# Weight splits moved from VectorE to GpSimd, with earlier refills and earlier high halves, in a linear attention and expert MLP kernel

## What is computed

```python
# attention, for every step t of every batch and head
y[:, :, t] = einsum('bhd,bhde->bhe', rt, state + (u * kt) outer vt)
state = wt[:, :, :, None] * state + kt outer vt
# MLP
h = maximum(x @ w_in, 0.0)
x = h * h @ w_out
# experts: tokens with x @ w_skip > 0 go to the expert with the highest logit
h = maximum(xc[mask] @ w1[e], 0.0)
y[mask] = gate_w[mask, None] * (h @ w2[e])
out[do_compute] = xc + y
```

## Time and profile before

| | us |
|---|---|
| median of 3 runs | 793.04 (792.3 to 793.43) |
| the profiled execution, its own time | 793.43 |
| its span | 791.7 |
| PE busy in the span | 759.2 |
| DVE / ACT / POOL busy | 468.3 / 323.9 / 224.9 |
| PE's chunk 0 in the trace | about 42.6 to 137.8 |

### The profile page before, as it was taken

How to read it: one execution, slowest core, us unless ns; L and a number is a source line. 1 busy time by engine, 2 the same in 40 slices (tenths; PEclk the granted TensorE clock), 3 DMA queues, 4 the chain that set the end, 5 groups by cost and what they waited for, 6 DMA issues and landing times.

```text
span 791.7 us, 15634 instructions
## 1 busy us (share of the span) xinstructions
PE 759.2 (96%) x5571; PEld 661.7 (84%) x5571; DVE 468.3 (59%) x755; ACT 323.9 (41%) x636; POOL 224.9 (28%) x215
## 2 busy tenths in 40 slices
PE   6699999999999999999999999999999999999994
PEld 3478788888888888888888889898889998999984
DVE  7876877766676665866576744344442246443861
ACT  3463443533344334433343333253342355353841
POOL 7842423222234220511242220253421002212210
PEclk9899999999999999999999999999999999999998
DMA  9874222422233223322231105155662116616520
GB/s 231 243 226 164 47 60 64 140 49 61 61 102 91 61 61 101 91 60 60 55 115 49 37 32 200 42 171 176 208 224 69 61 61 211 210 61 223 195 76 7
DMA packets 50420, 88.19 MB, mean 111 GB/s; under 512 B 5949, under 2 KB 33833, under 8 KB 50353
## 3 DMA queue, kind: packets, MB, share of 16 engines
q1 hardware_dynamic: 42192, 62.19, 28.1%
q0 software_dynamic: 7584, 24.31, 8.4%
q10 hardware_dynamic: 576, 0.79, 0.3%
HBM read 72.98 MB, written 16.75 MB: 113 GB/s over the span
## 4 chain that ended last, share of the span: by engine, by line
PE 82%; DVE 6%; DMA 4%; ACT 3%; issue 2%; POOL 1%; SPq 1%; DVEq 0%; POOLq 0%; ACTq 0%
PE bank L600 24%; PE bank L602 22%; PE bank L601 22%; DMA work<-sorted_rows 3%; PE bank L654 3%; PE bank L864 2%; PE bank L699 2%; PE bank L683 2%; ACT spare L968 1%; DMA work<-rkw 1%; PE bank L723 1%; PE bank L663 1%; PE bank L811 1%; DVE hid L1370 1%; DVE spare L1202 1%
## 5 line engine op out<-in xcount | busy, mean ns | idle before, releaser
L600 PE MATMUL bank<-wo_hi,h_hi 128*128 128x394 f32 (+1 forms) x576 | 201.8, 350 | 1.0 <-DVE h_lo L1491 1.0
L602 PE MATMUL bank<-wo_hi,h_lo 128*128 128x394 f32 (+1 forms) x576 | 196.6, 341 | 0.0
L601 PE MATMUL bank<-wo_lo,h_hi 128*128 128x394 f32 (+1 forms) x576 | 196.0, 340 | 0.0
L1370 DVE SCALAR_TENSOR_TENSOR hid<-bank,hid 128x512 f32<-128x512 f32 x96 | 65.1, 678 | 137.7 <-ACT hid L1011 137.7
L1011 ACT ACTIVATE hid<-bank 128x512 f32<-128x512 f32 x96 | 57.1, 594 | 158.0 <-PE bank L602 157.7
L600 PE MATMUL bank<-xt_hi,wi_hi 128*128 128x512 f32 x288 | 117.9, 409 | 0.1
L600 PEld LDWEIGHTS bank<-wo_hi,h_hi 128*128 128x128 f32 x576 | 108.7, 189 | 6.6 <-DVE h_lo L1491 1.2
L602 PE MATMUL bank<-xt_hi,wi_lo 128*128 128x512 f32 x288 | 112.9, 392 | 0.0
L601 PE MATMUL bank<-xt_lo,wi_hi 128*128 128x512 f32 x288 | 112.7, 391 | 0.0
L601 PEld LDWEIGHTS bank<-wo_lo,h_hi 128*128 128x128 f32 x576 | 108.8, 189 | 2.9
L602 PEld LDWEIGHTS bank<-wo_hi,h_lo 128*128 128x128 f32 x576 | 108.7, 189 | 0.0
(11 more groups left out here) (152 smaller groups left out, 1219.2 us busy)
## 6 DMA issues: line engine op xcount, KB each, us to landing
work<-rkw SPq DMA_DIRECT2D x48, 192.0 KB, 3.8
spare<-rk_rows SPq DMA_DIRECT2D x22, 384.0 KB, 4.2
work<-v_rows SPq DMA_DIRECT2D x25, 192.0 KB, 3.8
work<-sorted_rows SPq DMA_DIRECT2D x24, 193.0 KB, 2.6
work<-rkw SPq DMA_DIRECT2D x48, 96.0 KB, 3.3
x_cur<-sorted_rows SPq DMA_DIRECT2D x24, 192.0 KB, 2.4
work<-w POOLq DMA_DIRECT2D x6, 768.0 KB, 6.7
x<-w POOLq DMA_DIRECT2D x6, 768.0 KB, 9.7
```

Source lines behind the costliest of these rows:

```text
L600: pe.matmul(ps, a_hi, b_hi, start=start, stop=False, skip_group_check=True)
L601: pe.matmul(ps, a_hi, b_lo, start=False, stop=False, skip_group_check=True)
L602: return pe.matmul(ps, a_lo, b_hi, start=False, stop=stop, skip_group_check=True)
L1370: dve.scalar_tensor_tensor(hid[:, f % 2, :], HID[f % 2][:, :], 0.0, hid[:, f % 2, :], ALU.max, ALU.mult).then_inc(sb_sq, 1)
```

## The change

It has four parts. `keep_decay` moves from ACT to DVE, behind the scan that it reads, and the scans of units 2 to 4 no longer wait for it. The low halves of pieces 3 to 7 move from DVE to POOL: pieces 3 and 4 behind the factors of unit (1, 1), 5 and 6 behind those of (1, 2), 7 behind those of (1, 3). ACT's high halves of pieces 5, 6 and 7 stand one block earlier, at f = 6, 8 and 10. On SP, `refill(1, 2)` goes ahead of piece 6, and `refill(1, 3)` ahead of piece 7.

```diff
--- before.py
+++ after.py
@@ -281,7 +281,7 @@
         ROUTE_STEPS = 16
         LATE = 6
         SHORT = 7
-        SPLITS_AT = (1, 3, 5, 7, 9, 11)
+        SPLITS_AT = (1, 3, 5, 6, 8, 10)
         CHOICE_SLOT = 4
         GATE_SLOT = 12
         RANKS_UNIT = 2
@@ -499,11 +499,11 @@
             load_mlp_piece(4)
             load_transposed(2)
             load_mlp_piece(5)
+            refill(1, 2)
             load_mlp_piece(6)
             load_transposed(3)
+            refill(1, 3)
             load_mlp_piece(7)
-            refill(1, 2)
-            refill(1, 3)
             refill(2, 0)
             refill(2, 1)
             save_x2(0, 0)
@@ -1067,20 +1067,10 @@
                 act.wait_ge(ps_wg_turned, n + 1)
                 act.activation(wo_hi[:, 4 * n:4 * n + 4, DM:], gate_columns(n), ACT.Copy).then_inc(wg_hi, 1)
 
-            def keep_decay(b):
-
-                act.wait_ge(cum_done, b + 1)
-                act.activation(last_decay[0:PK, b, :].unsqueeze(2), by_time(cum[b % 2])[0:PK, :, T:T + 1], ACT.Copy
-                               ).then_inc(decay_saved, 1)
-
-            keep_decay(0)
             own_diagonal(0, 0)
-            keep_decay(1)
             for b in range(B):
                 if b == 1:
                     split_hi(0)
-                if b == 1 or b == 2:
-                    keep_decay(b + 1)
                 if b == 3:
                     take_gate(0)
                 take_k(0, b)
@@ -1175,10 +1165,14 @@
                     dve.wait_ge(r_done, unit - 1)
                 if not (isinstance(c, int) and unit <= B):
                     dve.wait_ge(sb_state, unit - 1)
-                elif unit >= 2:
-                    dve.wait_ge(decay_saved, unit - 1)
                 dve.tensor_tensor_scan(cum[n][0:PK], w_dec[n][0:PK], start_col[0:PK, :], 0.0,
                                        ALU.mult, ALU.add).then_inc(cum_done, 1)
+
+            def keep_decay(b):
+
+                dve.wait_ge(cum_done, b + 1)
+                dve.tensor_copy(last_decay[0:PK, b, :].unsqueeze(2), by_time(cum[b % 2])[0:PK, :, T:T + 1]
+                                ).then_inc(decay_saved, 1)
 
             def inverse(c, b, part):
 
@@ -1396,20 +1390,11 @@
                 dve.tensor_tensor(wo_lo[:, 4 * n:4 * n + 4, DM:], gate_columns(n),
                                   wo_hi[:, 4 * n:4 * n + 4, DM:].bitcast(F32), ALU.subtract).then_inc(wg_lo, 1)
 
-            def split_lo(k):
-
-                raw, hi, lo = mlp_piece(k)
-                dve.wait_ge(w_hi, k + 1)
-                dve.wait_ge(w_lo, k)
-                dve.tensor_tensor(lo, raw, hi.bitcast(F32), ALU.subtract).then_inc(w_lo, 1)
-
             def chunk(i, par, c, cg, c_last=False, late=0, per=8):
                 for f in range(NF):
                     square(i, f)
                     side(2 * f - late, c, cg, par, c_last, per)
                     square_lo(i, f)
-                    if isinstance(i, int) and i == 0 and f in SPLITS_AT[1:]:
-                        split_lo(2 + SPLITS_AT.index(f))
                     side(2 * f + 1 - late, c, cg, par, c_last, per)
                 for n in range(2 * NF - late, 2 * NF):
                     side(n, c, cg, par, c_last, per)
@@ -1437,9 +1422,11 @@
                 inverse(c, b, 1)
 
             decays(0, 0)
+            keep_decay(0)
             inverses(0, 0)
             own_term(0, 0)
             decays(0, 1)
+            keep_decay(1)
             inverse(0, 1, 0)
             mask_scores(0, 0, 0)
             mask_scores(0, 0, 1)
@@ -1448,6 +1435,7 @@
             for b in range(2):
                 take_xlo(0, 0, b)
                 decays(0, b + 2)
+                keep_decay(b + 2)
                 inverse(0, b + 2, 0)
                 mask_scores(0, b + 1, 0)
                 mask_scores(0, b + 1, 1)
@@ -1690,8 +1678,14 @@
             split_lo(1)
             keys(1, 0)
             split_lo(2)
-            for b in range(1, B):
-                factors(1, b)
+            factors(1, 1)
+            for k in (3, 4):
+                split_lo(k)
+            factors(1, 2)
+            for k in (5, 6):
+                split_lo(k)
+            factors(1, 3)
+            split_lo(7)
             for b in range(B):
                 factors(2, b)
```

## The result

The changed kernel takes **807.15 us** (median of 4 runs, 805.11 to 808.68), beside 793.23 us for the kernel before (4 runs, 792.3 to 793.77): a ratio of **1.0175, 95% interval [1.015, 1.02]**. It is slower, as forecast, but by 13.9 us instead of 5.1, and it lies 6 us above the top of the range. Run again on another chip it took 807.27 us. The profiled execution took 806.28 us, with a span of 804.6 us where before had 791.7.

What follows compares the result with a forecast made beforehand. PE, busy 759.2 of 791.7 us, was taken as the bound. Stall 3.9, removed wait -0.7, clock 1.7 and copies 0.2 sum to +5.1 us, giving 798.1 us; range 793.4 to 801.0.

Steps and rivals of the forecast that it cites:

- the delay beside POOL: Chunk 0, blocks 8 to 9: POOL's splits delay one DVE operation before `sb_state` by 0.8 us; bounds none and two.
- the clock: After PE's long wait before `k_transpose` of unit (1, 2), the granted clock falls once, costing 1.7 us; bounds 0 and 1.7.
- the step that carries the shift at the end of chunk 0 unchanged to the end: From chunk 1 on PE hardly waits, so chunk 0's shift reaches the kernel's end; nothing added later.
- The main term of the prediction: End of chunk 0: late piece 7 holds up ACT, moving `k_transpose` of unit (1, 2) 3.9 us later, from 105.35 to 109.3.
- Piece 6 and the other moves: Piece 6 lands at about 85.8, costing nothing; other moved halves cost nothing; `keep_decay` copies on DVE cost 0.2 us.
- the wait of 0.66 us at 115.35: PE's wait for `xt_lo` of unit (1, 2) in chunk 0 goes with DVE's split at 111.39, saving 0.7 us.
- What POOL adds: Chunk 0: low halves fit POOL's idle time but delay DVE once, 0.8 us, so `sb_state` reaches 6 at 96.3, not 95.5.
- This wait of 1.63 us goes: Chunk 0: without DVE's split at 86.52, `xt_lo` of unit (1, 1) is ready before PE arrives at 91.9.
- The new wait: Chunk 0: piece 7, issued at 99.0 behind `refill(1, 3)`, lands at 105.2; PE idles 6.4 us, `k_transpose` starts at 109.3.
- the mark of an error in its frame: Stated sign: the prediction is wrong in its frame if chunk 0's end shift is not that of the whole time.
- The rival of contention: Every two-SBUF-operand DVE operation on the way to `sb_state` pays 0.8 us, 2.4 in all: 799.7 us; chance 0.12.
- the fourth: Rival: piece 7 lands 8 us or more after issue, piece 6 is late, or another clock fall: 802 us; chance 0.06.

Runs made afterwards that it cites:

- piece7_at_11: The changed kernel with ACT's high half of piece 7 back behind block 11 instead of block 10, SP's new order kept; 800.84 us.
- sp_back: The changed kernel with SP's queue back in its old order, pieces 6 and 7 ahead of both refills; 798.02 us, ratio 1.0076.
- the measuring stretches: The kernel before with 28 and, in a second kernel, 24 trials ahead of it, timing DVE subtractions beside POOL's; the kernels' own times say nothing.
- after_again: The changed kernel run once more, unchanged, on the chip of the variants compared with it; 807.27 us.
- parts_of_512: The changed kernel with POOL subtracting each piece of `w_out` in three parts of 512 instead of four of 384; 807.51 us.
- piece5_early: The changed kernel with POOL subtracting piece 5 ahead of the factors of unit (1, 2) instead of behind them; 805.93 us.
- after_fill: The changed kernel with four useless operations on ACT and six on DVE ahead of the loops, restoring both programs' length; 803.23 us.

## Why the prediction was right, and where not

Three things of the sum failed: the delay beside POOL (0.8 us taken, 4.2 measured), the clock (one loss of 1.7 us taken, 4.7 to 5.0 in chunk 0), and the step that carries the shift at the end of chunk 0 unchanged to the end (chunk 3 adds 4.8 us, put at nothing).

**Right: the direction and the main chain.** The main term of the prediction is piece 7 behind `refill(1, 3)` with ACT's high half ahead of the ReLU of block 10; piece7_at_11 and sp_back both show it, each by undoing one end of the chain. "Piece 6 and the other moves" held: it was to land at about 85.8, and ACT's split of it starts at 85.73 (in a chunk 0 that began 1.0 us sooner, so it was 1 us later than worked out). `keep_decay` cannot be told from nothing, and the wait of 0.66 us at 115.35 went.

**Wrong in "What POOL adds": the delay beside POOL.** One delay of 0.8 us, bounded by none and two and looked for at block 9, was 4.2 us at block 8. The range of the term came from a single row beside a single form of group, and its mechanism (one instruction) is what the measuring stretches show, but not what `square_lo` of block 8 did. With it fell the step "This wait of 1.63 us goes": it became 3.7 us and brought a fall of the clock, 1.7 us, that the sum had not. `sb_state` reached 6 at 98.65, 2.3 us later than the 96.3 worked out and, counted from the start of chunk 0, as late as before the change. The stage hangs on that moment: DVE's relief never reached it.

**The new wait: the right chain, too early a place.** Issue 2.8 us after the refill's start (2.7 predicted). Landing 7.0 us after issue in this execution, and 6.5, 6.2, 6.2 and 6.2 in after_again, parts_of_512, piece5_early and piece7_at_11, against 6.2 predicted. So 2.3 us late by `sb_state` and 0.8 by the transfer: `k_transpose` at 112.48 for 109.3. PE's idle time of 5.36 us is shorter than the 6.4 predicted only because PE was late itself, by the wait before L742 and its clock. That the length came near is luck: two errors, a later landing and a later PE, all but cancel.

**Wrong in "The clock": one loss of 1.7 us.** Three falls, 1.7, 3.0 to 3.3 and 1.6 us. The bounds "0 and 1.7" took the price of a fall from one row, behind a wait of 2.29 us. Behind the wait of 5.36 us the lower level lasted about twice as long. The length of the wait alone does not set this: in parts_of_512 PE lost 1.9 us behind 7.05 (the granted clock was 0.51 from 115 to 119, then full), in after_fill 1.6 behind 4.45 (0.60 from 115 to 119). Nor does the row of 1.79 us at 56.19, from which the prediction took that a short wait costs nothing, hold in general: the same wait, 1.76 us at 57.50 in after_fill, is followed by 0.60 over 57 to 61.

**Missing: the code.** 4.8 us in chunk 3, from four instructions fewer on ACT and six fewer on DVE. "From chunk 1 on PE hardly waits, so a shift at the end of chunk 0 is carried to the end" was true of the trace of before and not of the changed program. None of the rivals had it. The prediction named this as the mark of an error in its frame: "if the shift at the end of chunk 0 is not that of the whole time" - it was 9.2 of 12.9.

Added up, the +5.1 us with `sb_state` 2.3 and the landing 0.8 us later, and 1.3 to 1.6 us more for the fall of the clock behind it, would be 9.5 to 9.8 at the end of chunk 0, where 9.2 was measured; the prologue, 1.0 us shorter in this execution, is in the 2.3 already. The rival of contention had the right direction, with 1.6 us more, and the fourth, at 802 us with 0.06, was the nearest to what happened.

## What to carry to other kernels

Ask of each operation that you want to take off a busy engine whether that engine is idle a few steps earlier or later: moving three splits within DVE's and ACT's own queues gained 0.5%, where moving DVE's to POOL and nothing else (splits_only) gained nothing that can be told. Look at what is queued behind the instruction that wants a transfer before you let it arrive late; one place further back hid 4 us of waiting. And when a loop far from the edit gets slower with waits that no semaphore ends, compare the packets of the instruction queue and pad the program ahead of the loop before looking for another reason.

## What the runs showed of the hardware

- The length of a program ahead of a loop is worth 4.8 us in the trace of the changed kernel (33 against 23 packets on the instruction queue, 3.2 us of PE waiting and 1.6 us of clock behind it), and 4.0 us between the medians of after_again and after_fill.
- A DVE subtraction with both operands in SBUF waits out an instruction of POOL of 2.75 us to its end. Beside short back-to-back ones it never waited for more than one of them in the 34 measuring trials in which they met. In eight of the traces of real kernels it waited for several, in seven beside parts of 384 (2.10 to 5.26 us for one `square_lo`) and in one beside parts of 512 (4.29 us); the reason is open.
- What a fall of the clock costs is not one number, and it does not follow the length of the wait: 1.7 us behind waits of 2.29 and 3.70 us, 1.6 behind 3.17 and 4.45, 3.0 to 3.3 behind 5.36, and 1.9 behind 7.05. A wait of 1.76 to 1.79 us left the clock full in before (56.19) and not in after_fill (57.50).
- A prologue that no edit touched differed by 2.6 us between two profiled executions, which hides a difference of that size in a single one.
